# Attention and two feed-forward layers on one core: the place of a block's end in the order of VectorE and ScalarE

## What is computed

```python
# 2 batches, 8 heads, 768 positions, head size 64; every query sees 96 local and 8 global keys
scores = scale * q @ k.T + bias, masked          # bias falls with the distance
x = softmax(scores) @ v                          # to (1536, 512)

h = x @ w_in1;  g = max(h, 0) + alpha * min(h, 0);  x = g @ w_out1       # 512 -> 2048 -> 512
h = x @ w_in2;  P = a0 + a1*h + a2*h**2 + a3*h**3
Q = 1 + |b0|*|h| + |b1|*h**2;  g = P / (Q + 1e-6);  out = g @ w_out2
```

## Time and profile before

| | us |
|---|---|
| median of three runs (lowest, highest) | 643.7 (642.78, 644.45) |
| the profiled execution | 645.31 |
| its span on the core | 643.6 |
| TensorE busy | 623.8 (97%) |
| VectorE busy | 436.1 (68%) |
| ScalarE busy | 319.7 (50%) |
| GpSimd busy | 286.1 (44%) |
| mean granted TensorE clock | 0.995 |

### The profile page before, as it was taken

One profiled execution on the slowest core, in us unless ns is written; L12 is line 12 of the kernel. 1 busy time (PEld: TensorE's weight loads), 2 busy tenths in 40 slices (PEclk: granted clock), 3 DMA queues, 4 the chain that ended last, 5 costly groups with the idle time before them and its releaser, 6 DMA issues.

```text
span 643.6 us, 9363 instructions
## 1 busy us (share of the span) xinstructions
PE 623.8 (97%) x3048; PEld 490.2 (76%) x3048; DVE 436.1 (68%) x721; ACT 319.7 (50%) x696; POOL 286.1 (44%) x239
## 2 busy tenths in 40 slices
PE   5989999999899999999999999999999999999996
PEld 4667777777677777778888888888888888888884
DVE  5856665555455656546555559988869988599885
ACT  5853444342233434322111167766668766677662
POOL 4767560000000000001444478887758767587772
PEclk9999999999899999999999999999999999999999
DMA  5781521111011111010322210000010000100001
GB/s 152 226 240 40 161 63 37 51 29 30 0 29 29 48 38 29 10 43 23 99 98 99 98 66 1 1 2 0 1 66 0 0 0 0 65 1 0 2 1 68
DMA packets 38677, 31.28 MB, mean 49 GB/s; under 512 B 8752, under 2 KB 33008, under 8 KB 38640
## 3 DMA queue, kind: packets, MB, share of 16 engines
q1 hardware_dynamic: 38640, 30.83, 15.6%
HBM read 27.67 MB, written 3.15 MB: 48 GB/s over the span
## 4 chain that ended last, share of the span: by engine, by line
PE 91%; DVE 3%; SPq 2%; ACT 1%; DMA 1%; issue 1%; POOL 1%; POOLq 0%; DVEq 0%; ACTq 0%
PE ps_h L593 31%; PE ps_y L626 20%; PE ps_y L628 19%; PE ps_o L593 5%; PE ps_s L593 5%; PE ps_w L543 3%; PE ps_o L564 2%; PE ps_o L553 2%; PE ps_y L508 1%; DMA kT<-in_k 1%; DVE g L1040 1%; SPq L399 1%; DVE g L1042 1%; DVE prob L1009 1%; PE ps_o L532 1%
## 5 line engine op out<-in xcount | busy, mean ns | idle before, releaser
L1258 POOL TENSOR_TENSOR win_lo<-stage,win_hi 128x1024 fp32r<-128x1024 f32 x8 | 19.2, 2402 | 226.4 <-DVE win_hi L1032 226.4
L593 PE MATMUL ps_h<-xy_hi,win_hi 128*128 (+1 forms) x288 | 116.3, 404 | 0.7 <-DVE xy_lo L978 0.7
L593 PE MATMUL ps_h<-xy_hi,win_lo 128*128 (+1 forms) x288 | 112.6, 391 | 0.0
L593 PE MATMUL ps_h<-xy_lo,win_hi 128*128 (+1 forms) x288 | 112.4, 390 | 0.0
L1056 DVE RECIPROCAL ps_h<-denom 128x512 f32<-128x512 f32 x24 | 80.6, 3360 | 17.3 <-POOL denom L1265 16.8
L1265 POOL TENSOR_TENSOR denom<-denom,q_abs 128x512 f32<-128x512 f32 x48 | 62.5, 1303 | 62.8 <-ACT denom L785 62.8
L626 PE MATMUL ps_y<-g_hi,wout_hi 128*128 128x512 f32 x192 | 79.3, 413 | 2.2 <-DVE xy_lo L1080 2.2
L1040 DVE TENSOR_SCALAR g<-ps_h,alpha_sb 128x512 f32<-128x512 f32 x48 | 36.0, 751 | 62.5 <-PE ps_h L593 62.5
L626 PE MATMUL ps_y<-g_hi,wout_lo 128*128 128x512 f32 x192 | 76.1, 397 | 0.0
L628 PE MATMUL ps_y<-wout_hi,g_hi 128*128 128x512 f32 x192 | 74.9, 390 | 0.0
L628 PE MATMUL ps_y<-wout_lo,g_hi 128*128 128x512 f32 x192 | 74.8, 389 | 0.0
(11 more groups left out here) (140 smaller groups left out, 1211.1 us busy)
## 6 DMA issues: line engine op xcount, KB each, us to landing
stage<-in_w_in SPq DMA_DIRECT2D x8, 512.0 KB, 3.3
stage<-in_w_out SPq DMA_DIRECT2D x8, 512.0 KB, 3.5
kT<-in_k SPq DMA_DIRECT2D x24, 128.0 KB, 2.3
vv<-in_v SPq DMA_DIRECT2D x24, 128.0 KB, 2.2
out<-xy_raw SPq DMA_DIRECT2D x12, 256.0 KB, 2.2
xy_raw<-in_w_in SPq DMA_DIRECT2D x4, 512.0 KB, 4.5
xy_raw<-in_w_out SPq DMA_DIRECT2D x4, 512.0 KB, 4.4
xy_raw_lo<-in_w_in SPq DMA_DIRECT2D x4, 512.0 KB, 4.6
```

The lines of the kernel that those rows point to most:

```text
L593: mm = pe.matmul(place, w[:, kc, cut], x[:, blk, kc, :], start=(kc == 0 and n == 0), stop=(kc == KC - 1 and n == 2))
L1258: pool.tensor_tensor(lo, raw, rounded, ALU.subtract).then_inc(w_ready, 1)
```

## The change

In a block with attention, the event `end` is yielded for the last m right after its `split`, ahead of the last two halves of the input product and the last `g`, instead of after the loop. Blocks without attention keep their order. Nothing else is changed.

```diff
@@ -314,12 +314,13 @@
                             yield what, s
                         yield "y", (m, half)
                     yield "split", m + 1
+                    if m == MC - 1:
+                        yield "end", None
                     for half in range(2):
                         for _, what, s in in_order(4 * m + 2 + half):
                             yield what, s
                         yield "h", (m + ahead, half)
                     yield "g", m + ahead
-                yield "end", None
                 return
             for m in range(MC):
                 made = m + ahead < MC or after is not None
```

## The result

The changed kernel takes 640.27 us in the median of six runs (638.89 to 641.7), the kernel before 643.27 us in six runs (641.65 to 644.76). The ratio is 0.9952, with a 95% interval from 0.9936 to 0.9968: 3.1 us less, between 2.1 and 4.1 (the medians themselves are 3.0 apart). The profiled execution took 640.21 us, with a span of 638.5. One execution of the kernel before, beside e5 to e8, took 776.48 us at a mean clock of 0.756, far from all others, and is left out of every count.

A forecast was written before the change was run, and what follows sets the result against it. TensorE, busy 623.8 of 643.6 us, was taken to bound the kernel, its longest wait being for VectorE's subtractions. 2.40 + 1.73 + 0.24 - 0.14 = 4.23 us off the 643.7 us median gave 639.5, range 638.4 to 641.6.

The forecast's parts named there:

- The hole: First end, TensorE between h(17) and the next output product: the whole standstill of 2.40 us goes.
- The clock term: First end, output product behind the standstill: its half-speed matmuls return to full clock, 1.73 us gained.
- The rival without the clock: No clock fall in the median run: late subtractions cost 0.41 us there, gain 2.9 us, time 640.8; chance 0.20.
- The wait before h(18): First end, TensorE's next input product waits for the later gate: a cost between 0 and 0.14 us, taken at 0.14.
- The second end: Middle block into the last: the output product finds all banks free, 0.24 us gained.
- The gain stays: Blocks after the first end keep their length (114.17 and 114.09 us); rival that it is given back, 643.7 us: 0.07.
- The clock elsewhere: Sign of a wrong prediction: in the profile after, the granted clock falls somewhere other than at the first end.
- The slower rival: Subtractions and copies collide in PSUM, TensorE stands 3.85 us before h(18): 1.2 us slower, 644.9; decides at 2.64 us; chance 0.03.

The follow-up runs named there:

- e5: Kernel before, with two of the four subtractions put ahead of the gate and two behind it, in both attention blocks; ratio to before 0.9956.
- e8: Changed kernel, with the first gate instruction of h(17) done twice instead of once at the first end; one execution, no ratio, stretch 244.87 us.
- e4: Changed kernel run again without any edit, as a second series; ratio to the kernel before 0.9929.
- e2: Changed kernel, but with the end early on VectorE in the first attention block only; ratio to the kernel before 0.9949.
- e3: Changed kernel, but with the end early on VectorE in the second attention block only; ratio to the kernel before 0.9997.
- e7: Changed kernel, with the first gate instruction of h(17) done five times instead of once at the first end; ratio to the kernel before 0.9985.
- e9: Kernel before, with the first gate instruction of h(17) done three times instead of once at the first end; ratio to before 1.0038.
- e1: Kernel before run again without any edit, twelve executions; ratio to before 0.9995.
- e10: Kernel before once more without any edit, one profiled execution; no ratio, stretch 247.78 us.

## Why the prediction was right, point by point

The forecast was 639.5 us, 4.2 us less, in a range from 638.4 to 641.6; measured are 640.27 and 3.1 less, then 4.6 less in e4. The mechanism is the one named. Term by term:

- **The hole, 2.40 us.** Right. It is 2.40 in all three profiles of the kernel before and zero in both of the changed one; e2 and e3 tie it to the first end.
- **The clock term, 1.73 us.** Right for the profiled execution, wrong as a constant. This is the term that was mis-sized, and the one that the prediction called unproven: the forecast added it in full, and gave the case without it 0.20. By the mean clocks it is there in some 45 of 70 executions. Neither case is the kernel: a single execution gains 4.50 us (with) or 3.25 (247.74 - 244.49, without), and the mean gain is 3.25 + 45/70 x 1.25 = 4.05 us, a ratio of 0.9937. Both measured intervals hold that value, the first one barely; taken alone, the first series (3.1 us) lies nearer to the rival (2.9) than to the forecast (4.2). That the sum of 4.23 is so near to 4.05 is in part luck: the clock term was 0.36 us too high in the mean (1.73 against 0.57 + 0.80), and the wait before h(18), below, took 0.14 us off that isn't there.
- **The rival without the clock.** It reckoned 0.41 us of waits for the banks, from the fourth subtraction alone. Measured are 0.57: the wait is 0.43, near what was worked out, and the restart behind it, which the rival left out, costs 0.1 us more. With that, the sum is 2.40 + 0.57 + 0.26 = 3.23 us, and the profiles say 3.25.
- **The wait before h(18), taken at 0.14 us.** Wrong; it is zero (169.54 to 172.26 is 2.72 us). The value was taken from the start of the first block, where it was no fixed cost either: in the changed kernel's profile the same place takes 2.73 us (50.00 to 52.73), and 0.14 had come with a split of 1.26 us on VectorE that now took 0.95. The gate, reckoned to end 0.54 us before h(18), ended 0.65 before it: the subtractions started 0.03 us after ScalarE's first copy instead of 0.1.
- **The second end, 0.24 us.** Right: 0.26 between the profiles, 0.26 in e2, 0.21 in e3.
- **The gain stays.** Right. From h(18) to the second h(17) are 114.07 us (172.26 to 286.33), as the 114.09 and 114.17 before.
- **The clock elsewhere.** The last fall, behind the last matmul, is in both kernels and costs TensorE nothing; it is no sign against the prediction, which had not seen it.
- **The slower rival.** Nothing of it happened: copies and subtractions overlap at their old lengths, 2.07 and 2.48 us for four. Its point of decision was right. It was put at a wait of 2.64 us with a fall; e7 made a hole of 2.64 us and came out 0.13 us from the kernel before.

Why the first series showed 3.1 us and the second 4.6 is not settled. Six runs of the changed kernel in each, with a prologue that varies by 2 us, a last part that varies by 1 us and, in the kernel before, a fall that comes or not, allow both.

The Trainium skill (TensorE: Matmul & The Clock Gate, section Part 1: The HAM clock gate) was named in the prediction for its sentence that the point of change differs from run to run. The runs agree: same kernel, same hole, 45 falls in 70 by the mean clock; and in the three profiles with a fall behind the hole, the granted clock falls 0.2 us (before), 0.05 us (e7) and 1.5 us (e9) after TensorE's restart. What the same section says of the default, that it is throttled and released by activity, shows here only with a delay: in e9 TensorE stands for 3.97 us, starts again at full pace, and is slow only from 174.69, 1.5 us later; and behind the last matmul of a run the fall takes 2.1 to 5.3 us to come.

## What to carry to other kernels

Where one engine's queue holds both work that a long product waits for and work that waits for that same product, the order decides: put first what is ready first. Here two instructions that could not run yet kept four that could behind them for 3.4 us, and moving them cost nothing as long as the displaced gate kept its 0.5 us of margin. Read a clock term from several executions before adding it to a sum, and compare profiles by a stretch that leaves out what varies between executions.

## What the runs showed of the hardware

- Whether TensorE's clock falls behind a standstill is a matter of the execution. It was rare in the runs with 1.5 us or less and frequent in those with 2.4 us or more: 1 of 21 executions with none or 0.3 us, none of 10 with 1.0, 1 of 6 with 1.5, 51 of 82 with 2.4, 5 of 10 with 2.6, 7 of 7 with 4.0. Within the longer ones the counts are too few to tell 2.4 from 4.0 us for certain. A mean clock of 0.996 or less was counted as a fall; in the six profiles with a hole of 2.4 us or more, it went with matmuls of 0.63 us behind the hole (before, e7, e9), and 0.997 or more with none (e1, e3, e10).
- In all three profiles with such a fall it came when TensorE was busy again, 0.05 to 1.5 us after the restart, and the granted clock was then 0.50 for 3.4 us (before, e7, e9). It came behind either of two places of the program (before y(0), before h(18)).
- Behind the last matmul of a run the clock falls in each of the twelve profiles, 2.1 to 5.3 us later. This and the 3.4 us above make up the mean clock: (2.9 + 3.4) x 0.5 / 643.6 = 0.005 for the 0.995 of the kernel before.
- A restart after a wait costs 0.1 us over the wait, in the distance between the first two matmuls (0.33 to 0.34 us instead of 0.23).
